# Attention, soft MoE and SoLU layer in one kernel: the first batch's order of loads, copies and transposes, and the place of eight small copies in the expert stage

## The reference, cut to what matters

```python
# 1 attention over pooled keys: 8 tokens are averaged, so 72 keys per head
k_p = k.reshape(B, H, Sp, pool, D).mean(axis=3)
v_p = v.reshape(B, H, Sp, pool, D).mean(axis=3)
scores = q @ k_p.T / sqrt(D);  attn = softmax(scores);  x = attn @ v_p
# 2 soft mixture of experts: x is (4608, 512), phi is (512, 32), 8 experts with 4 slots
logits = x @ phi
d = softmax(logits, axis=0);  slot_input = d.T @ x
slot_out[e] = relu(slot_input[e] @ w1[e]) @ w2[e]
x = softmax(logits, axis=1) @ slot_out
# 3 SoLU layer: h = x @ w_in (1024 columns), u = h * softmax(h), layer norm, @ w_out
```

## Time and profile before

| | us |
|---|---|
| median of 3 runs (lowest to highest) | 476.89 (476.36 to 479.6) |
| the profiled execution's own time | 478.42 |
| its span, first to last instruction | 476.6 |
| PE busy | 442.9 (93%) |
| DVE, ACT, POOL busy | 319.9, 253.8, 254.6 |
| HBM read, written | 66.13 MB, 9.44 MB |

### The profile page before, as it was taken

The page is one execution under the profiler, slowest core; times in us unless marked ns, Lnnn a source line. Parts: engine busy times, 40 slices in busy tenths (PEclk is TensorE's granted clock), DMA queues, the critical chain, the costliest instruction groups (busy, mean ns, idle before and its releaser), DMA issues.

```text
span 476.6 us, 9885 instructions
## 1 busy us (share of the span) xinstructions
PE 442.9 (93%) x3468; PEld 350.6 (74%) x3468; DVE 319.9 (67%) x534; ACT 253.8 (53%) x550; POOL 254.6 (53%) x346
## 2 busy tenths in 40 slices
PE   1897999999999998799859999999999999999996
PEld 0876888888888885344438887878788888888885
DVE  7655777768777774654557997767677777777411
ACT  2356567586766764303427765555556555555310
POOL 0396777888678522012114334656666666666540
PEclk9998899999999999999987999999999999999999
DMA  8969598988979564999900126666666666666652
GB/s 264 300 147 286 200 283 293 315 224 289 264 274 297 188 222 171 376 371 399 387 19 1 44 46 136 133 124 136 125 133 136 133 136 134 134 133 135 134 125 46
DMA packets 125342, 91.70 MB, mean 192 GB/s; under 512 B 104824, under 2 KB 104832, under 8 KB 123264
## 3 DMA queue, kind: packets, MB, share of 16 engines
q1 hardware_dynamic: 125312, 91.32, 69.6%
HBM read 66.13 MB, written 9.44 MB: 159 GB/s over the span
## 4 chain that ended last, share of the span: by engine, by line
PE 72%; SPq 12%; DVE 6%; DMA 3%; ACT 3%; issue 3%; POOL 1%; DVEq 0%
SPq L437 10%; PE banks L1442 9%; PE banks L1443 9%; PE banks L1444 9%; PE banks L1110 8%; PE banks L1162 5%; PE banks L1098 4%; PE banks L1178 3%; PE banks L1326 3%; PE banks L1142 3%; PE banks L1214 3%; PE banks L1346 3%; PE banks L1419 3%; PE banks L1186 2%; PE banks L1118 1%
## 5 line engine op out<-in xcount | busy, mean ns | idle before, releaser
L1442 PE MATMUL banks<-wo_hi,uh 128*128 128x512 f32 x288 | 112.8, 392 | 0.0
L1443 PE MATMUL banks<-wo_lo,uh 128*128 128x512 f32 x288 | 112.4, 390 | 0.0
L1444 PE MATMUL banks<-wo_hi,ul 128*128 128x512 f32 x288 | 112.1, 389 | 0.0
L545 POOL TENSOR_TENSOR ul<-u_col,uh 128x1024 fp32r<-128x1024 f32 x30 | 72.1, 2405 | 33.7 <-ACT uh L574 33.7
L471 POOL TENSOR_TENSOR attn<-attn,srec 128x576 f32<-128x576 f32 (+1 forms) x40 | 45.9, 1147 | 62.4 <-DVE srec L827 62.4
L760 ACT ACTIVATE sq<-u,usum 128x1024 f32<-128x1024 f32 x36 | 41.5, 1152 | 41.7 <-DVE u L1031 41.7
L1444 PEld LDWEIGHTS banks<-wo_hi,ul 128*128 128x128 f32 x288 | 54.2, 188 | 11.3
L1442 PEld LDWEIGHTS banks<-wo_hi,uh 128*128 128x128 f32 x288 | 54.2, 188 | 11.2
L1443 PEld LDWEIGHTS banks<-wo_lo,uh 128*128 128x128 f32 x288 | 54.2, 188 | 11.1
L1021 DVE TENSOR_REDUCE nmax<-banks 128x1 f32<-128x1024 f32 x36 | 43.5, 1219 | 18.5 <-PE banks L1419 18.4
L1110 PE MATMUL banks<-kblk,qT 128*128 128x144 f32 (+1 forms) x320 | 51.7, 309 | 4.5 <-issue 2.4
(11 more groups left out here) (158 smaller groups left out, 731.4 us busy)
## 6 DMA issues: line engine op xcount, KB each, us to landing
wslot<-in_moe_w SPq DMA_DIRECT2D x14, 2048.0 KB, 10.2
u_col<-u_blk SPq DMA_DIRECT2D x240, 64.0 KB, 2.1
qb<-in_q SPq DMA_DIRECT2D x32, 256.0 KB, 6.3
out<-osb SPq DMA_DIRECT2D x32, 256.0 KB, 2.5
kraw<-in_k SPq DMA_DIRECT2D x8, 640.0 KB, 7.9
vraw<-in_v SPq DMA_DIRECT2D x8, 640.0 KB, 5.2
kraw<-in_k SPq DMA_DIRECT2D x8, 512.0 KB, 6.3
vraw<-in_v SPq DMA_DIRECT2D x8, 512.0 KB, 4.0
```

The costliest lines, as they stand in the source:

```text
L545: pool.tensor_tensor(ul[par][:, :, :].rearrange("p c (q t) -> p (c q) t", q=4), v, uh[par][:, :, :].bitcast(F32).rearrange("p c (q t) -> p ...
L1442: pe.matmul(ps[4 + par], uh[par][:, c, :], wo_hi[:, c, :], start=(c == 0), stop=False)
L1443: pe.matmul(ps[4 + par], uh[par][:, c, :], wo_lo[:, c, :], start=False, stop=False)
L1444: last = pe.matmul(ps[4 + par], ul[par][:, c, :], wo_hi[:, c, :], start=False, stop=(c == FC - 1))
```

## The change

SP: the queries of batch 0's tile 2 are loaded right behind those of tile 1, ahead of g and of the keys of batch 1. PE: 30 transposes of the identity into an unused bank run before the first real work; the first scores wait for one more semaphore (`kT_upper`); `kT_t(1)` goes from step 2 to step 1 of batch 0. ACT: of the first six copies of keys it does four, DVE the other two, ahead of its folds of the values; ACT does `vT_close` of batch 0, behind `qT_evac` of tile 2; `kT_evac(1)` goes ahead of `lt_evac`, `exps` and `aT_evac` in step 2. DVE in the expert stage: `hz_evac(4)` to `hz_evac(7)` each go ahead of one or more of the `c4_lo` or `wo_low` beside them. `fold_piece` and `kblk_half` only name the operands that `both_halves` had in line.

```diff
+WARM = 30
...
-            load_q(0, 0, (1,))
+            load_q(0, 0, (1, 2))
             sp.dma_start(g8[:, :], g_v).then_inc(sem("g_in"), 16)
             sp.wait_ge(sem("k_pooled"), 1)
             load_k(1)
-            load_q(0, 0, (2, 3, 4))
+            load_q(0, 0, (3, 4))
...
+        def fold_piece(out, hh, g, a, n):
+            i = b_head[a * D:(a + 1) * D, g * P:(g + n) * P].rearrange(...)[:, hh]
+            if g == 2:
+                return out[:, :, 8 * POOL:SP], i[:, :, 0, 0::2]
+            return out[:, :, 4 * POOL * a:4 * POOL * (a + 1)].rearrange(...), i
...
             qT_evac((0, 0, 0))
-            kT_evac(0, 0)
+            act.wait_ge(sem("kT_ps"), 1)
+            for hh in range(2):
+                for g, n in ((0, 2), (2, 1)):
+                    o, i = fold_piece(kblk_half(0, hh), hh, g, 0, n)
+                    last = copy(o, i, 1.0 / POOL / D ** 0.5)
+            last.then_inc(sem("kT_sb"), 1)
             qT_evac((0, 0, 1))
             exps((0, 0, 0))
             vT_evac(0)
             qT_evac((0, 0, 2))
+            act.wait_ge(sem("vT_sb"), 1)
+            for hh in range(2):
+                c = V_LEFT + 1 + hh * HEAD
+                last = copy(vT[hh * D:(hh + 1) * D, :, :], vpad[hh * D:(hh + 1) * D, :, c:c + SP])
+            last.then_inc(sem("vT_closed"), 1)
             exps((0, 0, 1))
...
-                if t == 2 and not first and not last:
+                if t == 2 and not last:
                     kT_evac(b + 1, 1 - par)
...
                 aT_evac(tile, 1)
-                if t == 2 and first:
-                    kT_evac(b + 1, 1 - par)
...
             dve.wait_ge(sem("consts"), 1)
+            dve.wait_ge(sem("kT_ps"), 1)
+            for hh in range(2):
+                o, i = fold_piece(kblk_half(0, hh), hh, 0, 1, 2)
+                last = dve.tensor_scalar(o, i, 1.0 / POOL / D ** 0.5, None, ALU.mult)
+            last.then_inc(sem("kT_upper"), 1)
             for level in range(3):
                 fold(dve, "v", vraw, vp, 0, level)
...
             sub_max((0, 0, 1))
-            vT_close(0)
             vphi_evac(0, 0)
...
             hz_evac(3)
+            hz_evac(4)
             c4_lo(0)
-            hz_evac(4)
             c4_lo(1)
             wo_low(0)
+            hz_evac(5)
             c4_lo(2)
-            hz_evac(5)
             c4_lo(3)
             wo_low(1)
+            hz_evac(6)
             c4_lo(4)
-            hz_evac(6)
             wo_low(2)
             c4_lo(5)
+            hz_evac(7)
             c4_lo(6)
-            hz_evac(7)
             c4_lo(7)
...
             pe.wait_ge(sem("ident_ready"), 1)
+            for n in range(WARM):
+                pe.transpose(b_aT[0][:, 0:P], ident[:, :], ident[:, :])
             pe.wait_ge(sem("consts"), 1)
             qT_t((0, 0, 0), True)
             kT_t(0, True)
+            pe.wait_ge(sem("kT_upper"), 1)
             scores((0, 0, 0), True)
...
-                if t == (2 if first else 1) and not last:
+                if t == 1 and not last:
                     kT_t(b + 1)
```

More of the change, by code:

```diff
@@ L293, in c4_bank, with kblk_half @@
             return ps[5 + g % 2] if g < B else ps[7]
+        def fold_piece(out, hh, g, a, n):
+            i = b_head[a * D:(a + 1) * D, g * P:(g + n) * P].rearrange("p (g j h m) -> p h j g m", g=n, j=PAIRS, h=2)[:, hh]
+            if g == 2:
+                return out[:, :, 8 * POOL:SP], i[:, :, 0, 0::2]
+            return out[:, :, 4 * POOL * a:4 * POOL * (a + 1)].rearrange("p j (g m) -> p j g m", g=2), i
+        def kblk_half(par, hh):
+            return kblk[par][hh * D:(hh + 1) * D, :, hh * SP:(hh + 1) * SP]
         def dat_count(b, t):
@@ L586, in both_halves @@
                     for g, a, n in ((0, 0, 2), (0, 1, 2), (2, 0, 1)):
-                        i = b_head[a * D:(a + 1) * D, g * P:(g + n) * P].rearrange("p (g j h m) -> p h j g m", g=n, j=PAIRS, h=2)[:, hh]
-                        o = out(hh)[:, :, 4 * POOL * a:4 * POOL * (a + 1)].rearrange("p j (g m) -> p j g m", g=2)
-                        if g == 2:
-                            i, o = i[:, :, 0, 0::2], out(hh)[:, :, 8 * POOL:SP]
+                        o, i = fold_piece(out(hh), hh, g, a, n)
                         last = copy(o, i, scale)
@@ L594, in kT_evac @@
             def kT_evac(b, par):
-                both_halves("kT", b, lambda hh: kblk[par][hh * D:(hh + 1) * D, :, hh * SP:(hh + 1) * SP], 1.0 / POOL / D ** 0.5)
+                both_halves("kT", b, lambda hh: kblk_half(par, hh), 1.0 / POOL / D ** 0.5)
             def vT_evac(b):
```

## The result

The change makes the kernel faster: 470.33 us, the median of 4 runs (469.05 to 472.24), beside 476.62 for the kernel before (4 runs, 476.07 to 479.6). The ratio is 0.988, with a 95% interval of 0.985 to 0.991. The forecast was 471.7. The profiled execution took 472.24 us, of which 470.4 are span; the one before took 478.42. The difference is 6.2 us. Some executions are over 1.5% longer than the shortest of their kernel, at a lower granted clock; the ratios leave them out.

A forecast was written before the change was run, and what follows sets the result against it. PE, busy 93% of the span, was taken to pace the batches. Prologue 1.5, batch 1's keys 1.5, clock 1.0, second fall 0.4 and experts 0.75 sum to 5.15 us, taking the median from 476.89 to 471.7; range 468.0 to 475.5.

The forecast's parts named there:

- vT_close on ACT: Batch 0: ACT's two copies take 0.8 us in all, nothing waits for them; cost nothing, gain nothing.
- Keys of batch 0: Prologue: key copies done by 11.05, value folds slip 0.3, first scores at 11.65; tile 0's subtraction gains only 0.5 us.
- Queries of tile 2: Prologue: no wait for their load, transposes at 15.4, tile 1's scores at 16.25 instead of 17.45; gain 1.2 us.
- I count on the lower level again until about 26 us: Prologue: PE's waits from 8 to 14 us put its clock back to the lower level despite the 30 transposes.
- rival 1: The transposes keep the clock up through the prologue: 3.3 us more, 468.4 us; chance 0.15.
- 30 transposes: Kernel start: they take 6.6 us at the lower level, end at 8.6; cost nothing, other end 0.7 us.
- Keys of batch 1: Start of batch 1: idle of 2.36 us replaced by a stall of some 0.7; scores gain 1.5 us.
- The clock behind that gap: Batch 1's first scores: upper level expected, 1.2 us instead of 2.26; gain 1.0 us.
- The second fall: Clock fall at 48 us behind batch 1's thin matmuls: may stay; at most 1.7 us if avoided, 0.4 taken.
- Expert stage: Waits for hz at so_t(5) and so_t(6) go; gain 0.75 us through the last wo_low and copy of so.
- the transfers did not pace the batches: Against a rival: transfers pace the batches, an earlier start is used up waiting for queries, 0.75 left, 476.1 us; chance 0.06.
- the thin matmuls of later batches pulled nothing down: Against a rival: each batch's thin matmuls pull the clock down, up to 1.7 us in seven batches, 483.6 us; chance 0.05.

The follow-up runs named there:

- experiment 3: Kernel before with one edit, batch 0's tile 2 queries loaded right behind tile 1's: 475.85 us, ratio 0.999.
- experiment 7: Changed kernel with all six copies of batch 0's keys on ACT again: 472.26 us, ratio 0.993.
- experiment 1: Changed kernel without the 30 transposes: 471.4 us, ratio 0.987.
- experiment 2: Changed kernel with the queries of tile 2 loaded behind batch 1's keys as before: 475.62 us, ratio 0.995.
- experiment 6: Changed kernel with the transposes and copies of batch 1's keys in their old places: 472.95 us, ratio 0.990.
- experiments 5: Kernel before with two edits, tile 2's queries loaded early and vT_close of batch 0 on ACT: 473.72 us, ratio 0.993.
- experiment 12: Changed kernel with identity transposes added in PE's waits in the prologue, batch 0, the end of phase 1, the experts and the output stage: 466.16 us, ratio 0.978.
- experiment 8: Changed kernel with the expert stage's copies in their old order: 471.99 us, ratio 0.989.

## Why the prediction was right in its time, and where it was wrong

**The total** was sized 1.1 us short, 5.15 for 6.2, and the composition was further off than that, so the closeness of the total is in part luck. The steps:

- **vT_close on ACT: "Cost nothing, gain nothing". This step failed.** In the company of the rest it is worth 4.8 us by the ratios (0.998 with it undone, 0.988 with it), known to some 2 us; 4.2 by the two profiles at the first `hid_t`, of which 0.9 is a late first load. Alone it was not tried. The prediction read, rightly, that nothing waited for these copies in the kernel before. It did not ask what their 1.26 was made of. One such copy takes 0.30; 0.6 of the 1.26 was a wait for POOL's fold, so the end at 22.35 was pinned to the end of that fold, and with the fold where it was it could not come sooner. The thin matmuls ended at 22.66, only 0.3 later. What the early load won beyond that 0.3 would have stopped there, and in experiment 3 it did: the v72 transposes came 0.36 sooner.
- **Keys of batch 0: right for its place, nothing behind it.** DVE's copies took 0.30 each, for 0.27. The slip of the folds of 0.3 did not come: the copies were done at 10.64, not 11.05, since the transposes of the keys ahead of them began 0.2 sooner and ran at the upper clock (0.55 for 0.90), and the fold started at 10.68. The first scores came at 10.82, not 11.65. In the rows of experiment 7 the split carries nothing to batch 1.
- **Queries of tile 2: right, and more.** Their transposes began at 14.30 without a wait; 15.4 was forecast. The scores of tile 1 came 2.17 sooner instead of 1.2.
- **"I count on the lower level again until about 26 us": wrong.** In the profile after it was up for the transposes of the keys, down from about 12 us, and up again at about 15: the scores of tile 1 take 1.22, the thin matmuls 1.85. In six other profiles with the 30 transposes and the split it stayed up until 18 to 20 us, as rival 1 had it, and that alone won nothing, since PE waited for ACT and DVE. The speed of the thin matmuls came without the transposes in experiment 1 and by the early load alone in experiment 3, and experiment 2 loses it with the transposes in place. What goes with it is the wait ahead of tile 2's queries.
- **30 transposes: cost nothing.** Right; and taken out alone they gain nothing. They took 4.84 us, not 6.6. Together with the split they are worth about 0.7 by the traces.
- **Keys of batch 1: right.** 6.85 - 5.16 = 1.7 where 1.5 was forecast, 1.7 by experiment 6, with a stall of 0.80 for 0.7.
- **The clock behind that gap: right in size, the reason not shown.** 2.26 - 1.15 = 1.1 for 1.0. But experiments 5 and 6 kept the gap of 2.36 and their scores took 1.22 behind it; in experiment 6 the clock didn't fall at all there.
- **The second fall, 0.4: wrong.** It stayed, 3.4 us long. Its price, read in experiment 12, is 1.5 us.
- **Expert stage, 0.75: not borne out by any time.** With the new order alone the last `hid_t` came 0.15 sooner (231.15 - 231.00), for the weights were the bound there. At the copy of so the step holds as far as DVE goes: its last `wo_low` is done at 232.2 in the kernel after, and with the old order in experiment 8's kernel at 233.1. But the last `so_t` at the lower clock, 1.6 us longer, ended at 233.7 and used that up.

The sum by the trace: 5.2 up to tile 3's scores where 1.5 was forecast, 1.7 for 1.5, 1.1 for 1.0, which makes 8.0 at batch 1's thin matmuls; 0.7 of it is lost by the end of phase 1 (7.25), and 2.5 by the copy of so (238.56 - 233.77 = 4.8), where two pieces at the lower clock stand; the output stage gives 1.4 back, to 6.2, with less of its start at the lower clock (granted clock 0.82 from 244 to 262 us, 0.72 before). So the total was close because a gain of 3.7 that was not foreseen met losses that were not foreseen either, and both depend on where the clock fell: with the fall at 19 us the first gain is 1.7 to 2.4. Of the rivals, the transfers did not pace the batches (PE waited for no load from 60 to 170 us) and the thin matmuls of later batches pulled nothing down (window of 60 to 80 us at 1.00).

What stays open is why PE's clock falls at one seam in one run and not in the next. The falls in the prologue, at batch 1's thin matmuls, at the first `hid_t` and at the last `so_t` come and go between kernels that are the same there, and each costs up to 2 us; that is also what limits the verdicts above.

## What to carry to other kernels

When an operation looks harmless because nothing waits for it, compare its duration with the shortest of its kind in the trace: a copy that takes twice its least may itself be waiting for something, and then its end will not move when the work before it does. Two edits can stand in for each other, like the transposes and the split here: undone one at a time, each looks worthless. A change in one engine's order should be priced together with the work that stands just behind the wait, because the early load alone brought nothing and its partner, read in the timeline of before, looked like nothing. Cheap transposes of the identity in PE's waits, 97 more in experiment 12 from the prologue to the output stage, brought about 1% together; which of them pay was not taken apart. At the kernel's start, ahead of waits, undoing them changed nothing. And one profile's clock is one draw: compare a stretch over all profiles that share its code before giving it a price.

## What the runs showed of the hardware that was not expected

Two VectorE copies within SBUF, 0.31 us each by themselves, took 1.26, 2.83 and 3.23 us together beside a GpSimd instruction of 2.9 us: the first lasted until 0.2 us behind that instruction's end, whenever it had started, and the second took 0.31. VectorE's subtraction from PSUM (0.76) and its row sums within SBUF (0.75) took their usual time beside the same instruction, and ScalarE did the two copies in 0.89 beside it. GpSimd's instruction was not slowed (2.89 to 2.90 in all).

The granted clock in the windows reads 1.00 ahead of its first recorded change: in the kernel before the stretches from 10.4 to 17.2 us and from 17.2 to 20.0 show 1.00 while eight score matmuls take 2.26 in the one and 2.13 in the other, against 1.22 at 28.71. Early in a kernel the durations tell the level, not that column.
